# Attention and two mixture-of-experts layers on one core: the first share column and y additions placed among what is left of the first unit, and the early x sums spread over attention steps

## What is computed

```python
logits = x @ w_gate
P = np.exp(logits - logits.max())
for _ in range(8):
    P /= P.sum(1, keepdims=True) + 1e-09
    P /= P.sum(0, keepdims=True) + 1e-09
    P *= N / E
for e in range(E):
    h = np.maximum(x @ w1[e], 0.0)
    ye = h @ w2[e]
    out += P[:, e:e + 1] * ye
```

## Time and profile before

| | us |
|---|---|
| median of 3 timed runs | 1413.57 |
| lowest and highest of them | 1413.27, 1424.87 |
| the profiled execution | 1407.47 |
| its span, first to last instruction | 1405.6 |
| mean granted TensorE clock in it | 0.977 |
| PE busy | 1346.3 (96% of the span) |
| PE busy in each of the 17 stretches of 50 us from 250 to 1100 us | 50.00, at a granted clock of 1.00 |
| DVE busy | 854.0 |
| ACT busy | 538.8 |

### The profile page before, as it was taken

The page is one execution under the profiler, slowest core; times in us unless marked ns, Lnnn a source line. Parts: engine busy times, 40 slices in busy tenths (PEclk is TensorE's granted clock), DMA queues, the critical chain, the costliest instruction groups (busy, mean ns, idle before and its releaser), DMA issues.

```text
span 1405.6 us, 21176 instructions
## 1 busy us (share of the span) xinstructions
PE 1346.3 (96%) x7802; PEld 1215.0 (86%) x7802; DVE 854.0 (61%) x1898; ACT 538.8 (38%) x940; POOL 95.4 (7%) x112
## 2 busy tenths in 40 slices
PE   8999799999999999999999999999999965999997
PEld 5887688999998889999888999988899845889997
DVE  5559766656666665686666656666666446886000
ACT  5776233333343333353333333343333112444421
POOL 5651000000000000000000000000000000102101
PEclk9999899999999999999999999999999985999999
DMA  8751011111122111112211111122112014775530
GB/s 187 183 144 62 30 61 60 60 60 60 60 92 87 60 60 60 60 61 75 105 60 60 60 60 60 63 104 71 60 60 75 31 45 138 259 258 167 190 107 23
DMA packets 92569, 125.57 MB, mean 89 GB/s; under 512 B 37216, under 2 KB 43360, under 8 KB 92512
## 3 DMA queue, kind: packets, MB, share of 16 engines
q1 hardware_dynamic: 90464, 118.53, 25.8%
q0 software_dynamic: 2048, 6.29, 1.5%
HBM read 118.52 MB, written 6.29 MB: 89 GB/s over the span
## 4 chain that ended last, share of the span: by engine, by line
PE 88%; DVE 6%; ACT 2%; issue 1%; POOL 1%; DMA 1%; SPq 0%; DVEq 0%; POOLq 0%
PE PS L1561 23%; PE PS L1563 23%; PE PS L1562 23%; PE PS L1860 6%; PE PS L1843 5%; PE PS L1693 2%; DVE G L1467 1%; PE PS L1674 1%; PE PS L1664 1%; PE PS L1890 1%; ACT sc L711 1%; DVE hlo L1160 1%; PE PS L1539 1%; DVE w1lo L1005 0%; PE PS L1818 0%
## 5 line engine op out<-in xcount | busy, mean ns | idle before, releaser
L1561 PE MATMUL PS<-xhi,w1hi 128*128 128x384 f32 x896 | 301.5, 336 | 5.2 <-ACT h_sum L758 4.2
L1563 PE MATMUL PS<-xhi,w1lo 128*128 128x384 f32 x896 | 300.8, 336 | 0.0
L1562 PE MATMUL PS<-xlo,w1hi 128*128 128x384 f32 x896 | 300.7, 336 | 0.0
L1561 PE MATMUL PS<-w2hi,hhi 128*128 128x512 f32 x744 | 291.8, 392 | 7.6 <-DVE acc L1168 4.7
L1562 PE MATMUL PS<-w2lo,hhi 128*128 128x512 f32 x744 | 291.7, 392 | 0.0
L1563 PE MATMUL PS<-w2hi,hlo 128*128 128x512 f32 x744 | 291.6, 392 | 0.0
L1170 DVE SCALAR_TENSOR_TENSOR acc<-PS,prob_e,acc 128x512 f32<-128x512 f32 x180 | 134.9, 750 | 162.6 <-PE PS L1563 162.6
L738 ACT CAST w2hi<-raw 128x2048 fp32r<-128x2048 f32 x31 | 59.3, 1912 | 372.6 <-PE PS L1563 372.6
L1561 PEld LDWEIGHTS PS<-xhi,w1hi 128*128 128x128 f32 x896 | 169.0, 189 | 7.9 <-ACT h_sum L758 4.5
L1561 PEld LDWEIGHTS PS<-w2hi,hhi 128*128 128x128 f32 x744 | 140.8, 189 | 37.0 <-DVE acc L1168 5.2
L1562 PEld LDWEIGHTS PS<-xlo,w1hi 128*128 128x128 f32 x896 | 169.1, 189 | 1.2
(11 more groups left out here) (237 smaller groups left out, 1607.9 us busy)
## 6 DMA issues: line engine op xcount, KB each, us to landing
raw<-in_w SPq DMA_DIRECT2D x64, 1024.0 KB, 5.6
expert_weights<-in_w SPq DMA_DIRECT2D x10, 2048.0 KB, 11.6
raw<-in_w SPq DMA_DIRECT2D x3, 2048.0 KB, 8.0
first_expert_w<-in_w SPq DMA_DIRECT2D x3, 2048.0 KB, 14.4
vs<-in_v SPq DMA_DIRECT2D x16, 192.0 KB, 3.1
x_rows<-acc SPq DMA_DIRECT2D x2, 1536.0 KB, 7.9
vw<-in_v SPq DMA_DIRECT2D x16, 120.0 KB, 3.0
qs<-in_qT SPq DMA_DIRECT2D x4, 384.0 KB, 3.8
```

What stands on the lines that cost most here:

```text
L1561: T.matmul(o, whi, xh, start=first, stop=False, skip_group_check=shared)
L1562: T.matmul(o, whi, xl, start=False, stop=False, skip_group_check=shared)
L1563: return T.matmul(o, wlo, xh, start=False, stop=last, skip_group_check=shared)
```

## The change

Behind the Sinkhorn steps DVE now makes the share column of expert 0, and then takes the six y additions of unit 0 with the ten remaining operations between them: one `h_lo`, one `h_lo`, one `w1_sums`, two `w1_lo`, two `w1_lo`, none, and the last three `w1_lo` at the end. `layer1` no longer makes them for the first expert of the first chunk. In attention the four early `x_sums` move from step 44 to steps 44, 45, 46 and 47, one in each; `x_hi` begins one step later (44 in place of 43), and so does `x_lo` (46 in place of 45). No operation and no transfer is added or removed.

```diff
@@ attend_window of ACT @@
-                    if STEPS - 5 <= s < STEPS - 5 + PARTS:
-                        x_hi(0, s - (STEPS - 5), True)
+                    if STEPS - 4 <= s < STEPS - 4 + PARTS:
+                        x_hi(0, s - (STEPS - 4), True)
@@ attend_window of DVE @@
-                    if s == STEPS - 4:
-                        for n in range(SUMS):
-                            x_sums(0, n, True)
-                    if STEPS - 3 <= s < STEPS - 3 + PARTS:
-                        x_lo(0, s - (STEPS - 3), True)
+                    if STEPS - 4 <= s < STEPS - 4 + SUMS:
+                        x_sums(0, s - (STEPS - 4), True)
+                    if STEPS - 2 <= s < STEPS - 2 + PARTS:
+                        x_lo(0, s - (STEPS - 2), True)
@@ layer1 of DVE @@
-                else:
-                    prob_column(c, i)
-                    for _ in y_adds(c, i, 0, True):
-                        pass
@@ behind the Sinkhorn steps, DVE @@
+            prob_column(0, 0)
+            first_ys = y_adds(0, 0, 0, True)
+            for n in (1, 1, 1, 2, 2, 0):
+                next(first_ys)
+                for _ in range(n):
+                    next(aside, None)
             for _ in aside:
                 pass
```

## The result

The timed executions of before and after, 12 each, have medians of 1414.7 us (1410.08 to 1428.38) and 1405.7 us (1402.81 to 1409.48): 9.0 us less. The ratio is 0.9907 with an interval of 0.9879 to 0.9935, which is 9 to 17 us less. The profiled executions took 1407.47 and 1403.55 us, only 3.9 us apart. So one question is answered (the kernel is faster, by under 2%), and two are open: why the profiles differ by less than the 8.5 us of the sum, and the ratio by more.

The account below looks back on a forecast made before the run. PE carries 88% of the chain that ended last, so only its waits and half clock count. Gains of 7.7 + 0.8 = 8.5 us against the median 1413.57 gave 1405.1 us, range 1398 to 1412.

Parts of the forecast that it names:

- the sum: Whole kernel: 7.7 us from the column and additions plus 0.8 from the x sums, 8.5 us gain, bounds 4.9 to 10.5.
- Part 1: Unit 0's products: share column and y additions earlier on DVE remove 4.9 us of PE waiting and 2.8 of half clock, 7.7.
- rival C: DVE's queue, 164 to 177 us: additions hold `w1_lo` so long that unit 2 starves, 2.4 us slower, 1416.0; chance 0.03.
- Rival A: Unit 0's products: the stall goes but the half clock stays, gain 5.7 us, 1407.9; chance 0.10.
- Part 2: Attention, steps 44 to 47: one x sum per step shifts PE 1.5 us earlier, DVE's pace keeps 0.8; bounds 0 and 1.5.
- the rival's 180.8: Follow-up with only the x sums spread: TensorE's shift lasts in full, Sinkhorn end at 159.4, unit 2 at 180.8; no chance given.
- Rival D: PE's whole 1.5 us shift stays and the clock recovers sooner at both remaining stalls: gain 11.8 us, 1401.8; chance 0.06.
- the two stretches: Half clock of 5.28 and 3.15 us behind stalls that stay: may differ by up to 2.6 us, 1.3 of time either way.
- The lower bound of 4.9: Low end of the whole gain, 4.9 to 10.5 us; also the products' gain if the half clock comes all the same.
- The range: Time of the whole kernel: low 1398, high 1412 us, with the 6.1 us between profiled execution and timed median taken as spread.
- B: Unit 0: the wait for addition 0 ends as late as before, only the x sums' gain stays, 1412.8 us; chance 0.06.

Follow-up runs that it names:

- part 1 alone: Only the share column and six y additions moved, x sums in the old order, against the kernel before: 1401.75 us median, ratio 0.9927.
- part 2 alone: The kernel before with only the x sums, `x_hi` and `x_lo` spread as in the change: 1406.42 us median, ratio 0.9938.
- the kernel before once more: The kernel before, nothing changed, timed and profiled again: 1418.08 us median, ratio 0.9995.
- the run with the burst back: The changed kernel plus three unused VectorE additions (1.4 us) behind the x sum of step 44: 1402.76 us median of 11, ratio 0.9961.
- the changed kernel once more: The kernel with the whole change, nothing else altered, timed and profiled again: 1398.46 us median, ratio 0.9882.

## Why the prediction was right, point by point

The forecast was 1405.1 us and the median 1405.7; the likeliest gain was 8.5 us and the measured one 9.0 by medians. The steps fare better than the total, which was partly luck.

**Part 1, 7.7 us.** Right in its size and its reason. The stretch of the products fell by 7.77 us in the profile after, and took the same 16.36 us in the runs of part 1 alone and of both changed kernels. The margins were as forecast: no addition made TensorE wait. The price of the rival C, the order behind waiting additions, was real: 5.6 us when the ten stand behind all six, as in the earlier trace rows VectorE lets nothing pass. The slack of 3.8 us for the first `w1_lo` is what the chosen order keeps.

**Rival A** (the half clock stays) fell: the clock was 1.00 through the products. In the one profile with a wait of 2.69 us at this place it was 1.00 as well.

**Part 2, 0.8 us.** The mechanism in the profile was right: the scores of step 45 came at 103.97 (forecast 103.86), TensorE's wait fell to 0.15 us, the first full x sum came at 117.95 (forecast 117.86), and the restart in unit 1 was 0.90 us earlier, at 144.29 against 145.19. One more run gave VectorE 1.2 us of work more and found the restart in unit 1 later by as much, which is the pace that the step assumed. Unit 2 began at 173.90, where 173.8 was forecast. The run of part 2 alone had unit 2 at the rival's 180.8, helped by a shorter half-clock stretch, so the 0.8 us rest on the rows of VectorE and not on unit 2.

**What the step missed.** I put the 1.6 us wait down at its own length. The sum counted half clock in one profile only and held the attention clear of it. In other executions of the kernel before, the clock falls behind this short wait and stays at half for up to 14 us. The two profiles that show 14 us (the kernel before once more, and part 1 alone) were both some 10 us late at unit 2. The timed executions have no trace, but each has its mean granted clock. Of the 80 executions of the kernel before in the experiments (without the one of 2267.3 us), 47 took 1404.8 to 1411.2 us, all at 0.975 to 0.980, and 33 took 1415.7 to 1425.2, all at 0.962 to 0.974. So the slower level goes with a lower clock; that the clock fell at this wait in each of them is inferred from the profiles and from the run with the burst back. The levels lie 10.5 us apart by their means, so with 33 in 80 part 2 is worth some 4.3 us more on average, and 8.5 + 4.3 = 12.8 us is inside the measured 9 to 17. It can't be told more exactly, because the share of slower executions differs from one set of executions to the next: 16 of 25, 9 of 29, 3 of 17, 5 of 9.

**Where luck came in.** The profiled execution gave a second forecast, 1399.0 for its own successor. The first profile after took 1403.55, but the changed kernel once more took 1398.18 to 1399.0. The first twelve executions of the changed kernel lie 4 to 11 us above these four. The six fastest of them, 1402.81 to 1404.48, had the same mean clock (0.979 to 0.981, against 0.978 to 0.981), so the clock does not explain their 4 to 6 us; the one with a trace lost 4.4 us in the second layer. The twelve executions of before have their fastest at 1410.08, 5.3 us above the fastest of the 80. Something seems to have made both kernels some 5 us longer in that first set. It drops out of the difference, and the forecast of 1405.1 took it over with its base, the median 1413.57. What it was isn't shown.

**Slips in the working.** They don't touch the forecast itself. Rival D takes the 2.6 us of the two stretches in full, where the sum rightly takes half, 1.3; it should read 10.5 us and 1403.1. The lower bound of 4.9 leaves out the same 1.3 that the upper one has, and should be 3.6. The scores of step 45 work out at 102.93 + 0.89 = 103.82, not 103.86. The 16 and 7 matmuls of the earlier trace rows come from two places of one profile, so they say nothing of one run against another; the later runs do. And the trace has more than three stretches of half clock: another of 41 us lies in the second layer, from 1147.2 us on, with TensorE busy for half of it. All 13 profiles have it, 41 to 44 us long, so it adds nothing to the difference.

**The range** held. Its argument, that the profiled execution and the median of before lie 6.1 us apart, could have been a sign that executions of this kernel differ by more than the sum allowed; the prediction took it as spread and did not ask where the 6.1 us were.

**Rivals B, C and D** as stated did not come. D's "clock recovers sooner" is seen, but as a spread of both signs: from the restart behind the 4.2 us wait to full clock it took 3.05 to 5.93 us over the runs.

## What to carry to other kernels

A short wait of TensorE ahead of a dense stretch can cost several times its length in part of the executions (1.6 us of waiting and some 10 us of time here), so one profile doesn't price it; look at how the timed executions and their mean clocks cluster, and profile twice. When operations are put between waiting ones on an in-order engine, work out for each when it is wanted and when its place in the queue comes: the same ten operations cost nothing between the additions, 3.0 us behind the first and 5.6 us behind all. And a lump of work ahead of a consumer's first release (four x sums) is worth moving behind the releases when its own user comes much later: that gave 4.7 us more here.

## What the runs showed of the hardware

I had not expected TensorE to stay at a granted clock of 0.50 for some 14 us while it was busy all the time (74 matmuls from 109 to 124 us at 0.54 on average), when behind longer waits it was back at full clock after 3.0 to 6.1 us. Nor that a wait of 1.5 to 1.6 us in a stretch of short matmuls is followed by half clock in three of four profiles, while one of 2.69 us among matmuls of 512 columns is not in its one profile, and one of 2.82 to 2.83 us among the same matmuls is in all ten profiles that have it. Behind the same wait of 4.2 to 4.3 us, full clock was back 3.05, 3.64, 4.44, 4.64, 5.28 and 5.93 us after the restart in different runs. The Trainium skill, "TensorE: Matmul & The Clock Gate", Part 1, says that the number of half-clock matmuls at a kernel's start varies from run to run. These differ likewise, behind a wait within the kernel. Half of such a difference is time, since a matmul takes twice as long at half clock (0.43 against 0.23 us from start to start at 512 columns), so a gain of under 1.4 us can't be read off one profile behind such a stall.
